# Order of SP's queue, ScalarE's copies and VectorE's low parts in the first tile of a fused attention and MLP kernel, and two sums of v moved to VectorE

## The chip, the cores and the metric

The kernel runs on one core of a Trainium2 chip. The metric is the device time of one execution in microseconds. Of three runs before the change the median is 788.79 us (787.68 to 790.22). A core has five engines with a queue each: TensorE (PE, matmuls and transposes), VectorE (DVE), ScalarE (ACT), GpSimd (POOL) and SyncE (SP), which here only issues DMAs. Each engine runs its queue in order; between engines there are only semaphores.

## The reference, cut to what matters

```python
q, k, v: (4, 8, 576, 64)                     # float32
q_d, k_d, v_d = means of 4 neighbouring rows # 144 pooled rows
out_d    = softmax(scale * q_d @ k_d.T) @ v_d
out_up   = repeat(out_d, 4, axis=2)
mask     = |i - j| < 4
out_local = softmax(where(mask, scale * q @ k.T, -1e9)) @ v
x = (out_up + out_local) as (2304 tokens, 512)
x = (x @ w_a) * (x @ w_b) @ w_out            # 512 -> 1536 -> 512
h = x @ w_in                                 # 512 -> 1024
solu = h * softmax(h)
y = layernorm(solu) * g_ln @ w_out2          # 1024 -> 512, the output
```

All is float32. Each product of the two MLPs is done as three matmuls on split operands: a high part (the value rounded by a copy to the type fp32r) and a low part (the value minus the high part): high x high, low x high, high x low.

## The kernel before, in words

The 2304 tokens are six tiles of 384. Tile m's block j (12 blocks of 128 of the 1536 middle columns) is: two up-products (kinds WA and WB, `up_product`, 12 matmuls each) of block j+1, and one down-product of block j (`down_product`, 12 matmuls into four PSUM banks that stay open through the tile). g = 12m + j counts blocks through all tiles. Between the products lie 36 gaps a tile, n = 3j, 3j+1, 3j+2 (`between(m, n)` exists on TensorE, ScalarE and VectorE): attention for tile m+1 is done in them piece by piece. `jobs_at` places the pooled attention: job i has scores at its first gap (`pooled_scores`), maximum on VectorE a gap later, exponentials on ScalarE two gaps later, a transposition three later (`turn_pooled`, copied by ScalarE's `pT_copy`), values four later (`pooled_values`, copied and stored by `out_d_copy`). In tile 0 job 0 starts at gap 0, job 1 at gap 5, so its values are due at gap 9. `local_at` places the local attention on VectorE: 17 steps a unit (7 products and reductions of q and k, the softmax, then products with v and sums; ScalarE does four of the v-parts, `unit_values`) and an END step, which writes `accT`; two units a tile, (1,0) and (1,1) in tile 0. `turns_at` places the four transpositions of the finished x (`turn_x`), in tile 0 at gaps 29, 30, 32 and 33. `QK_AT` places the pooling of raw q (gap 15) and raw k (gap 17) of the next batch, 48 small matmuls each.

What a block passes through: TensorE up(g,A) -> ScalarE `a_copy(g)` -> VectorE `gate(g)` once up(g,B) is done -> ScalarE `ab_high(g)` -> VectorE `ab_low(g)` (GpSimd in tiles 4 and 5) -> TensorE down(g). up(g,B) also needs gate(g-1), as they share a PSUM bank. W_out's block needs, in tile 0 and up to block 6 of tile 1, a DMA into one of three slots (`load_wo(g)`, free once down(g-3) is done), ScalarE's `wo_high(g)` and `wo_low(g)` (VectorE for blocks 0 and 1, GpSimd after). The weights W_a and W_b come in pairs of blocks (`load_weights(i)`, blocks 2i and 2i+1) and need ScalarE's `weight_high(j)` and `weight_low(j)` (VectorE for blocks 0 and 1, GpSimd after) in tile 0.

Ahead of tile 0 is the head: attention for tile 0 with nothing to hide it, for four pairs c of heads, on all engines: `head_local(c)` copies the local part to `x_raw`, `head_turn_pooled(c)` and `head_up(c)` do the pooled part, `head_x(c)` adds them, `x_high`, `x_low` split them. v_d, the pooled v of batch 0, comes from `raw_v` by `pool_v` on GpSimd, two additions of halves each, for the pairs in the order 1, 2, 3, 0. Then VectorE does the low parts of the first two blocks and the first two local steps, and `gate(0)`.

What sets the order around the change: every engine's queue is written out by hand, so an instruction that waits holds up all behind it. SP's queue (from `load_q_head` to `tile(m)`) issues nearly all DMAs; `tile(m)` puts loads at blocks j or gaps n, and many wait for semaphores first. `load_unit_v(1, 0)` overwrites `raw_v`, so it waits for all sums of v.

## Time and profile before

| | |
|---|---|
| median of 3 runs | 788.79 us (787.68 to 790.22) |
| the profiled execution | 785.7 us |
| its span, first to last instruction | 783.9 us |
| mean granted TensorE clock | 0.991 of full speed |
| TensorE busy | 762.2 us, 97% of the span |
| VectorE busy | 549.0 us, 70% |
| ScalarE busy | 299.0 us, 38% |
| GpSimd busy | 193.3 us, 25% |

Busy time is that of instructions on the engine; idle time of an engine matters only where another waits for it. The waits of an engine are listed with the instruction that released it; a wait for several semaphores goes to the one that came last, and "issue" is a wait of which the profile shows no releaser. Times are counted from the span's start. Matmuls overlap, so each shows about 0.33 us while they start 0.17 apart.

### The profile page before, as it was taken

How to read it: one execution, taken by the hardware profiler on the slowest of the kernel's cores; microseconds unless marked ns; L12 is line 12 of the kernel's file. 1: busy time of each engine (PE TensorE's matmuls, PEld its weight loads, DVE VectorE, ACT ScalarE, POOL GpSimd, SP SyncE). 2: the span in 40 equal slices, each digit the busy share in tenths (PEclk: the TensorE clock that was granted, in tenths of full speed). 3: DMA queues.
4: the chain of work that ended last, by engine and by line, in shares of the span. 5: the costliest groups of instructions: out<-in, count | busy, mean ns of one | idle time of the engine just before them, and what ended most of it. 6: DMA issues, size and time to landing. Idle time of an engine off the chain costs nothing.

```text
span 783.9 us, 12654 instructions
## 1 busy us (share of the span) xinstructions
PE 762.2 (97%) x4626; PEld 706.4 (90%) x4626; DVE 549.0 (70%) x978; ACT 299.0 (38%) x819; POOL 193.3 (25%) x244
## 2 busy tenths in 40 slices
PE   8997899898999999999999999999999999999998
PEld 7886899898999999999999999999988888888886
DVE  6796777979869887778777776122467766666663
ACT  4644537363353534344524424234322222222222
POOL 3656655355414330050001111122100000000000
PEclk9998999999999999999999999999999999999999
DMA  9999946586788575572746433636121011011011
GB/s 183 219 208 203 215 136 184 154 260 181 227 208 231 143 212 172 161 216 80 218 140 177 139 94 111 206 104 216 53 68 54 27 54 54 28 54 54 29 41 40
DMA packets 94650, 108.84 MB, mean 139 GB/s; under 512 B 29309, under 2 KB 62589, under 8 KB 94589
## 3 DMA queue, kind: packets, MB, share of 16 engines
q1 hardware_dynamic: 83293, 99.38, 48.3%
q10 hardware_dynamic: 11296, 8.65, 3.5%
q8 instruction: 37, 0.61, 0.3%
q14 instruction: 24, 0.20, 0.1%
HBM read 87.46 MB, written 20.55 MB: 138 GB/s over the span
## 4 chain that ended last, share of the span: by engine, by line
PE 91%; SPq 5%; DMA 1%; issue 1%; DVE 1%; ACT 0%; DVEq 0%; ACTq 0%
PE psum L931 28%; PE psum L933 27%; PE psum L932 27%; PE psum L1058 2%; SPq L503 2%; PE psum L888 2%; PE psum L841 1%; PE psum L865 1%; PE psum L899 1%; SPq L532 1%; DMA wo_raw<-in_moe_w_out 1%; PE psum L875 1%; SPq L557 1%; DMA v_h<-in_v 1%; SPq L469 1%
## 5 line engine op out<-in xcount | busy, mean ns | idle before, releaser
L931 PE MATMUL psum<-x_hi,w_hi 128*128 128x384 f32 x576 | 198.8, 345 | 0.6 <-DVE x_lo L1467 0.4
L933 PE MATMUL psum<-x_hi,w_lo 128*128 128x384 f32 x576 | 193.7, 336 | 0.0
L932 PE MATMUL psum<-x_lo,w_hi 128*128 128x384 f32 x576 | 193.5, 336 | 0.0
L1477 DVE TENSOR_TENSOR ab_f<-psum,a_sb 128x384 f32<-128x384 f32 x72 | 39.9, 554 | 104.4 <-PE psum L933 62.6
L931 PEld LDWEIGHTS psum<-x_hi,w_hi 128*128 128x128 f32 x576 | 109.0, 189 | 3.7 <-issue 3.3
L932 PEld LDWEIGHTS psum<-x_lo,w_hi 128*128 128x128 f32 x576 | 108.9, 189 | 0.0
L933 PEld LDWEIGHTS psum<-x_hi,w_lo 128*128 128x128 f32 x576 | 108.7, 189 | 0.0
L931 PE MATMUL psum<-ab_hi,wo_hi 128*128 128x384 f32 x288 | 100.9, 350 | 4.5 <-issue 4.5
L933 PE MATMUL psum<-ab_hi,wo_lo 128*128 128x384 f32 x288 | 97.7, 339 | 0.0
L932 PE MATMUL psum<-ab_lo,wo_hi 128*128 128x384 f32 x288 | 97.5, 339 | 0.0
L1817 POOL TENSOR_TENSOR ab_lo<-ab_f,ab_hi 128x384 fp32r<-128x384 f32 x24 | 29.5, 1229 | 182.6 <-ACT ab_hi L1229 182.6
L1510 DVE TENSOR_TENSOR tmp<-q_u,k_u 128x768 f32<-128x768 f32 x70 | 69.4, 994 | 3.7 <-DMA k_u<-in_k 3.6
L1224 ACT ACTIVATE a_sb<-psum 128x384 f32<-128x384 f32 x72 | 35.1, 487 | 85.4 <-PE psum L933 81.7
L1791 POOL TENSOR_TENSOR raw<-raw 96x256 f32<-96x256 f32 x42 | 40.4, 989 | 105.7 <-DMA raw<-in_q 49.9
L1519 DVE TENSOR_REDUCE p_u<-tmp 128x12 f32<-128x768 f32 x70 | 66.0, 942 | 0.1
L1229 ACT ACTIVATE ab_hi<-ab_f 128x384 fp32r<-128x384 f32 x72 | 37.5, 521 | 65.5 <-DVE ab_f L1477 59.5
L931 PEld LDWEIGHTS psum<-ab_hi,wo_hi 128*128 128x128 f32 x288 | 54.9, 190 | 6.9 <-issue 6.7
L1259 ACT ACTIVATE e_sb<-psum,neg_max 128x1024 f32<-128x1024 f32 x18 | 20.1, 1118 | 106.3 <-DVE neg_max L1681 106.3
L1869 POOL TENSOR_TENSOR rstd<-var_eps,exponent 128x1 f32<-128x1 f32 x18 | 9.9, 550 | 194.4 <-DVE var_eps L1703 194.4
L931 PE MATMUL psum<-w_hi,lnT_hi 128*128 128x512 f32 x144 | 57.6, 400 | 0.0
L933 PE MATMUL psum<-w_hi,lnT_lo 128*128 128x512 f32 x144 | 56.3, 391 | 0.0
L931 PE MATMUL psum<-win_hi,y_hi 128*128 128x512 f32 x144 | 56.1, 390 | 0.0
(157 smaller groups left out, 1427.6 us busy)
## 6 DMA issues: line engine op xcount, KB each, us to landing
wo_hi<-wo_hi_scratch SPq DMA_DIRECT2D x53, 256.0 KB, 2.7
wo_lo<-wo_lo_scratch SPq DMA_DIRECT2D x53, 256.0 KB, 3.1
wo_raw<-in_moe_w_out SPq DMA_DIRECT2D x19, 256.0 KB, 4.7
yT_scratch<-y_sb ACTq DMA_DIRECT2D x6, 768.0 KB, 5.9
y_raw<-yT_scratch SPq DMA_DIRECT2D x18, 256.0 KB, 2.9
out<-out_sb SPq DMA_DIRECT2D x18, 256.0 KB, 2.1
k_u<-in_k SPq DMA_DIRECT2D x11, 384.0 KB
v_u<-in_v SPq DMA_DIRECT2D x11, 384.0 KB
```

Source lines behind the costliest of these rows:

```text
L503: sp.dma_start(paired_rows(t)[:, :, x, :], bass.AP(src.tensor, b * H * S * D + half * 3 * R4 * D + x * PPB * S * D, [[6 * R4 * D, PPB * BL ...
L931: mm(dst, wh, xh, start=first, stop=False, skip_group_check=not check)
L932: mm(dst, wh, xl, start=False, stop=False, skip_group_check=not check)
L933: last = mm(dst, wl, xh, start=False, stop=end, skip_group_check=not check)
L1224: A(a_sb[:, g % 2, :], bank(GA, NT), ACT.Copy).then_inc(s.a_copied, 1)
L1229: A(ab_hi[:, g % 2, :], ab_f[:, g % 2, :], ACT.Copy).then_inc(s.ab_hi_ready, 1)
L1259: A(e_sb[:, par, :], psum[:, HB[par][0] * BANK:HB[par][0] * BANK + F2], ACT.Exp, bias=neg_max[:, par:par + 1], accum_out=e_sum[:, par:par ...
L1477: V.tensor_tensor(ab_f[:, g % 2, :], bank(GB, NT), a_sb[:, g % 2, :], ALU.mult).then_inc(s.ab_ready, 1)
L1510: last = V.tensor_tensor(tmp[:, step % 3], q_u[:, :, :], k_u[:, :, step * D:step * D + TPP * D], ALU.mult)
L1519: last = V.tensor_reduce(p_u[:, step - 1, :], tmp[:, (step - 1) % 3] .rearrange("p h (t d) -> p (h t) d", d=D), AX.X, ALU.add)
L1791: last = G.tensor_tensor(t[:, :, i, 0:128], t[:, :, i, 0:128], t[:, :, i, 128:256], ALU.add)
L1817: G.tensor_tensor(ab_lo[:, g % 2, :], ab_f[:, g % 2, :], ab_hi[:, g % 2, :], ALU.subtract).then_inc(s.ab_lo_by_pool, 1)
```

## The change

In words, by engine:

- SP: after `load_unit_v(1, 0)`, which now waits for two sums of GpSimd and two of VectorE, `load_weights(3)` and `load_wo(3)` are issued ahead of raw q (they were in tile 0's block 1). `load_weights(4)` and `(5)` go to blocks 2 and 4, behind `load_wo` of the block; unit (1,1)'s q and k go from gap 11 to 9, its v from gap 19 to 16; the store of pooled v and the load of raw k go from block 3 to gap 10; `load_vd(1)` from gap 10 to 13.
- VectorE: `sum_v(1)` and `sum_v(0)`, two reductions each, in the head; the head's last steps interleaved in another order; in all tiles `ab_low(g)` ahead of the gap 3j; in tile 0 the local steps of gaps 16 on run faster and end at gap 27 rather than 29.
- ScalarE: `weight_high(0)` ahead of `head_pooled_pT(2)`; in all tiles `a_copy(g+1)` ahead of gap 3j+1, and `wo_high(g+1)` behind gap 3j+2; in tile 0 `weight_high` by the table `SPLIT_AT`, blocks 8 and 9 in j = 6, 10 and 11 in j = 7.
- GpSimd: `pool_v` for pairs 2 and 3 only; `weight_low` by the same table.
- TensorE: `head_turn_pooled(3)` ahead of `head_up(1)`; waits on sums of v split by who makes them.

```diff
--- before.py
+++ after.py
@@ -97,8 +97,8 @@
         if m == 0:
-            todo = 2 * STEPS - FIRST
-            first, end = FIRST + n * todo // 30, FIRST + (n + 1) * todo // 30
+            first, end = (FIRST + i * 16 // 15 if i < 16 else 19 + (i - 16) * 4 // 3 for i in (n, n + 1))
         else:
@@ -108,6 +108,9 @@
+SPLIT_AT = {0: (2,), 2: (4,), 3: (5,), 4: (6,), 5: (7,), 6: (8, 9), 7: (10, 11)}
...
@@ -596,8 +599,11 @@
-            sp.wait_ge(s.v_summed, PPB)
+            sp.wait_ge(s.v_summed, 2)
+            sp.wait_ge(s.v_by_vector, 2)
             load_unit_v(1, 0)
+            load_weights(3)
+            load_wo(3)
             load_raw(1, 0, 0)
@@ -606,24 +612,19 @@
                         store_wo(g)
-                    if m == 0 and j in (1, 3, 5):
-                        load_weights((j + 5) // 2)
-                    if m == 0 and j == 3:
-                        store_vd(1, 0)
-                        store_vd(1, 1)
-                        load_raw(1, 1, 0)
-                        load_raw(1, 1, 1)
-                    if g + SLOTS - 1 < FC * TILES and (m > 0 or j > 0):
+                    if g + SLOTS - 1 < FC * TILES and (m > 0 or j > 1):
                         load_wo(g + SLOTS - 1)
+                    if m == 0 and j in (2, 4):
+                        load_weights(j // 2 + 3)
                     for n in range(3 * j, 3 * j + 3):
...
                             rest = m in (0, 3)
-                            if n == (11 if m == 0 else 4):
+                            if n == (9 if m == 0 else 4):
                                 load_unit_q(m + 1, 1)
...
                                 load_xup(m + 1, 0)
-                            if n == (19, 14, 14, 20, 14)[m]:
+                            if n == (16, 14, 14, 20, 14)[m]:
                                 load_unit_v(m + 1, 1)
@@ -650,7 +651,12 @@
             def pooling(m, n):
-                if (m, n) in ((0, 10), (3, 10)):
+                if m == 0 and n == 10:
+                    store_vd(1, 0)
+                    store_vd(1, 1)
+                    load_raw(1, 1, 0)
+                    load_raw(1, 1, 1)
+                if (m, n) in ((0, 13), (3, 10)):
                     load_vd(1 if m == 0 else 3)
@@ -807,8 +813,10 @@
                     pe.wait_ge(s.raw_v_loaded, 32)
+                elif c == 1:
+                    pe.wait_ge(s.v_by_vector, 1)
                 else:
-                    pe.wait_ge(s.v_summed, c)
+                    pe.wait_ge(s.v_summed, c - 1)
                 if c == 0:
@@ -879,7 +887,8 @@
                 if JOBS[i][3] == 0:
-                    pe.wait_ge(s.v_summed, PPB)
+                    pe.wait_ge(s.v_summed, 2)
+                    pe.wait_ge(s.v_by_vector, 2)
                 else:
@@ -1029,8 +1038,8 @@
             head_turn_pooled(2)
+            head_turn_pooled(3)
             head_up(1)
-            head_turn_pooled(3)
             head_up(2)
@@ -1292,8 +1301,8 @@
             head_pooled_exp(3)
+            weight_high(0)
             head_pooled_pT(2)
-            weight_high(0)
             head_pooled_pT(3)
@@ -1308,14 +1317,15 @@
                     between(m, 3 * j)
-                    if m == 0 and j != 1 and j + HEAD_BLOCKS < FC:
-                        weight_high(j + HEAD_BLOCKS)
-                    between(m, 3 * j + 1)
+                    if m == 0:
+                        for i in SPLIT_AT.get(j, ()):
+                            weight_high(i)
                     if g + 1 < FC * TILES:
                         a_copy(g + 1)
+                    between(m, 3 * j + 1)
+                    between(m, 3 * j + 2)
                     if g > 0 and g + 1 < FC * TILES and wo_fresh(g + 1):
                         wo_high(g + 1)
-                    between(m, 3 * j + 2)
                     if g == 0:
@@ -1439,6 +1449,15 @@
+            def sum_v(c):
+                dve.wait_ge(s.raw_v_loaded, 32)
+                for x in range(2):
+                    last = V.tensor_reduce(v_d[:, c, x, :].rearrange("p (y d) -> p y d", y=2),
+                                           raw_v[:, x, :, c, :].rearrange("p y (r d) -> p y d r", r=R4),
+                                           AX.X, ALU.add)
+                last.then_inc(s.v_by_vector, 1)
             def head_local(c):
@@ -1502,7 +1521,8 @@
-                        dve.wait_ge(s.v_summed, PPB)
+                        dve.wait_ge(s.v_summed, 2)
+                        dve.wait_ge(s.v_by_vector, 2)
                         dve.wait_ge(s.q_loaded, 16 * loads_to(u, 0, TPP))
@@ -1632,22 +1652,24 @@
             head_pooled_max(3)
-            head_local(3)
+            sum_v(1)
             head_pooled_norm(2)
             head_pooled_norm(3)
+            head_local(3)
             head_x(0)
+            weight_low(0, WA)
             head_x(1)
-            weight_low(0, WA)
             x_low(0, 0)
             head_x(2)
+            x_low(0, 1)
             head_x(3)
-            x_low(0, 1)
-            weight_low(0, WB)
             x_low(0, 2)
             x_low(0, 3)
+            weight_low(0, WB)
             wo_low(0)
...
                 weight_low(1, kind)
+            sum_v(0)
             wo_low(1)
@@ -1656,9 +1678,9 @@
                     g = FC * m + j
-                    between(m, 3 * j)
                     if m < LOW_BY_POOL:
                         ab_low(g)
+                    between(m, 3 * j)
                     between(m, 3 * j + 1)
@@ -1834,7 +1856,7 @@
                 normalise(c)
-            for i, c in enumerate((1, 2, 3, 0)):
+            for i, c in enumerate((2, 3)):
                 pool_v(i, c)
@@ -1843,8 +1865,9 @@
                         ab_low(g)
-                    if m == 0 and 2 <= j < FC - HEAD_BLOCKS:
-                        weight_low(j + HEAD_BLOCKS)
+                    if m == 0 and j > 1:
+                        for i in SPLIT_AT.get(j, ()):
+                            weight_low(i)
                     if g > 0 and g + 1 < FC * TILES and wo_fresh(g + 1):
```

## Rows read from the trace of the kernel before

**Rows 1.** The page, busy us of each engine, its share and instructions.

```profile
PE 762.2 (97%) x4626; PEld 706.4 (90%) x4626; DVE 549.0 (70%) x978; ACT 299.0 (38%) x819; POOL 193.3 (25%) x244
```

**Rows 2.** TensorE's waits, 0 to 180: total us, times, longest us.

```profile
PE psum L888 <- ACT pT_pool L1155: 5.4, 1, 5.4
PE psum L899 <- DVE accT L1574: 2.6, 1, 2.6
PE psum L931 <- issue: 2.4, 1, 2.4
...
PE psum L825 <- ACT pT_head L1138: 1.0, 1, 1.0
```

**Rows 3.** Windows: length, busy of each engine (instructions), clock, DMA share, GB/s.

```profile
37.70:49.20 11.50, 11.12 (x72) 10.36 (x71) 11.50 (x18) 5.60 (x12) 3.47 (x5) 1.00 1.09 199
...
66.70:89.80 23.10, 15.28 (x89) 14.88 (x90) 15.69 (x13) 12.11 (x36) 16.20 (x19) 0.85 0.96 193
89.80:141.40 51.60, 51.60 (x363) 49.30 (x361) 38.39 (x53) 26.74 (x68) 29.70 (x33) 1.00 0.60 161
```

**Rows 4.** TensorE's timeline: start, us, line, tiles; in brackets idle before it.

```profile
47.10 0.33 PE L931 MATMUL psum<-x_hi,w_hi 128*128 128x384 f32 x1
...
49.18 0.33 PE L931 MATMUL psum<-ab_hi,wo_hi 128*128 128x384 f32 x1
...
184.41 0.41 PE L931 MATMUL psum<-ab_hi,wo_hi 128*128 128x384 f32 x1 [2.13 <-issue]
...
185.36 0.52 PE L933 MATMUL psum<-ab_hi,wo_lo 128*128 128x384 f32 x1
```

**Rows 5.** Chain of waits, pieces in order: start us, us, what.

```profile
73.86 0.32 PE psum L932
...
76.10 0.23 PE psum L933
...
144.53 0.32 PE psum L931
...
147.74 0.26 PE psum L932
```

**Rows 6.** ScalarE's timeline.

```profile
34.28 1.04 ACT L1203 ACTIVATE w_hi<-w_raw 128x1024 fp32r<-128x1024 f32 x1
...
70.95 0.63 ACT L1208 ACTIVATE wo_hi<-wo_raw 128x512 fp32r<-128x512 f32 x1 [8.36 <-DMA wo_raw<-in_moe_w_out]
```

**Rows 7.** SP's timeline of DMA issues; last, raw q from issue to landing.

```profile
47.43 13.07 SPq L503 DMA_DIRECT2D raw<-in_q  x4
...
64.20 1.08 SPq L541 DMA_DIRECT2D wo_raw<-in_moe_w_out  x2
...
84.73 1.72 SPq L557 DMA_DIRECT2D q_u<-in_q  x4
...
DMA to landing us min/median/max: 6.2/10.6/14.3
```

**Rows 8.** VectorE's groups, 66 to 142: busy us, mean ns, idle before.

```profile
L1550 DVE TENSOR_TENSOR tmp<-v_u,p_u 128x768 f32<-128x768 f32 x6 | 8.7, 1464 | 0.0
...
L1519 DVE TENSOR_REDUCE p_u<-tmp 128x12 f32<-128x768 f32 x7 | 6.6, 944 | 0.1
```

**Rows 9.** VectorE's timeline.

```profile
44.71 0.94 DVE L1519 TENSOR_REDUCE p_u<-tmp 128x12 f32<-128x768 f32 x1
45.57 0.54 DVE L1477 TENSOR_TENSOR ab_f<-psum,a_sb 128x384 f32<-128x384 f32 x1
...
61.98 3.01 DVE L1535 TENSOR_SCALAR u_den<-u_sum 128x12 f32<-128x12 f32 x1
...
86.43 1.07 DVE L1481 TENSOR_TENSOR ab_lo<-ab_f,ab_hi 128x384 fp32r<-128x384 f32 x1
...
182.00 2.31 DVE L1481 TENSOR_TENSOR ab_lo<-ab_f,ab_hi 128x384 fp32r<-128x384 f32 x1
```

**Rows 10.** GpSimd's timeline.

```profile
73.03 3.85 POOL L1791 TENSOR_TENSOR raw<-raw 96x256 f32<-96x256 f32 x3
```

More of the change, by code:

```diff
@@ L385, in build_program @@
         names = w_names + wo_names + wos_names + raw_names + qh_names + kh_names + """v_h_loaded q_loaded k_loaded v_loaded
-        xup_loaded xup_stored0 xup_stored1 raw_v_loaded v_step v_summed vd_stored0 vd_stored1 vd_loaded y_stored win_loaded w2_loaded g_loaded y_loaded0
+        xup_loaded xup_stored0 xup_stored1 raw_v_loaded v_step v_summed v_by_vector vd_stored0 vd_stored1 vd_loaded y_stored win_loaded w2_loaded g_loaded y_loaded0
         y_loaded1 out_stored0 out_stored1
```

## The prediction, made before the changed kernel ran

> **What bounds the kernel now.** The page first: TensorE is busy 762.2 of 783.9 us [rows 1], so whatever is not on its path is free, and only about 22 us of the span, plus slow-clock time, can be won at all. So the second view is the table of what TensorE waited for, up to 180 us. It has four entries that matter [rows 2]: 5.4 us for `pT_pool`, a copy by ScalarE; 2.4 us put down to "issue"; 2.6 us for `accT`, an addition by VectorE; 1.0 us for `pT_head`. The timeline adds a fifth of 2.13 us in tile 1, at 184.41 [rows 4]. All five lie in stretches whose order the change rewrites. Below, tile 0's block j is up-products for block j+1 (kinds A and B), then down-product j; n = 3j, 3j+1, 3j+2 are the gaps.
>
> The third view is the windows. From 66.70 to 89.80 TensorE is busy 15.28 of 23.10 us at a mean granted clock of 0.85, and at 1.00 from 89.80 to 141.40, where it never stops [rows 3]. At full speed (2.4 GHz) the twelve matmuls of up(1,B), 47.10 to 49.18, take 2.08 us, 0.173 each [rows 4]. The first window holds up(4), down(3), up(5), down(4): 24+12+24+12 = 72 matmuls, 12.5 us, and the sixteen small ones of pooled_values (0.65 at full speed, as at 53.89). So 23.10 - 13.15 = 9.95 us are lost there: 5.43 and 2.40 in waits, 2.1 in matmuls at the 1.2 GHz level after the long wait (0.32 apart until 76.10 [rows 5]).
>
> The fourth view names the cause. ScalarE sits 8.36 us before `wo_hi` at 70.95, released by the DMA of `wo_raw`; `pT_pool` comes right behind it at 71.49 [rows 2, 6]. That DMA is W_out of block 3, issued only at 64.20, because SP spent 47.43 to 60.50 issuing raw q and then the weights [rows 7]. So TensorE waits for a copy that needs nothing from W_out, and only stands behind it in ScalarE's order.
>
> **The change part by part** (minus is faster).
>
> 1. Head. weight_high(0), 1.04 us at 34.28 [rows 6], stands before the copy `pT_head` that TensorE waits 1.0 for [rows 2]; now it runs in ScalarE's idle time of 2.17 us ahead of 33.9. Then, in VectorE's new order with its own durations (1.1 for a norm, 0.5 for local, head_x and x_low, 0.6 for a w_lo or wo_lo, start to start): norm(3) done at 33.4, local(3) 33.9, head_x(0) 34.4, w_lo(0,WA) 35.1, and by turns head_x and x_low until the last x_low at 38.7. TensorE, with turn(3) ahead of up(1), is through the head's ups at 36, so up(0,A) ends near 39.3 where it ended at 41.9. But the next gate belongs to VectorE, which is busy without a break there, and two sum_v are added. Price of sum_v: not in this trace. Bounds: two reductions of 512 input elements; the nearest row is 944 ns for 768 [rows 8], so 0.63 each; from below 1.15 a pair, since the next instruction starts 0.86 after such a reduction (44.71 to 45.57 [rows 9]); from above 2.0, if they are slowed as products beside GpSimd are (1464 against 944 [rows 8]). I take 1.25, by the reductions' own row. sum_v(1) fills a 1.2 us hole; sum_v(0) is on the path. From 38.7 VectorE has w_lo(0,WB), wo_low(0) and two w_lo of block 1, to 41.1; sum_v(0), 42.3; wo_low(1), 42.9; two products and a reduction, 2.7, so gate(0) stays at 45.6 to 46.05 [rows 9]: what it saved in the head, it adds. up(1,B) needs that gate: it starts at 46.1 instead of 47.10. Gain 1.0 of the 2.6; the rest becomes a wait of 1.8 us there, the size after which the clock sometimes fell for some ten matmuls (2.13 at 184.41 did it, 2.4 at 85 did not); half of 1.5: +0.8. Bounds of the head: -2.5 to +1.5.
> The Trainium skill (SBUF — State Buffer, section "Who interferes with whom") says that a VectorE instruction with two SBUF inputs contends with a GpSimd instruction that reads SBUF, and a tensor_reduce never does. By that rule sum_v keeps the lower price beside GpSimd's own sums, and the sum stands; without it 0.75 is added for sum_v(0). The 944 against 1464 agrees.
>
> 2. The wait of 5.43. pT_copy(1) goes ahead of wo_high(3); weights 3 and W_out 3 go ahead of raw q in SP's queue. Weights 3 issue from 47.4, W_out 3 waits for down(0), now at 50.2, and lands near 62.5 rather than 70.95. pT_copy(1) then needs only the turn at 63. The wait goes, and with it the slow clock.
>
> 3. The wait of 2.40 at 87.60. VectorE's ab_lo of block 4 runs at 86.43 for 1.07 [rows 9], behind a local step, and down(4) starts as it ends. Now ab_low(g) precedes the steps. The wait goes. So 2 and 3 give 9.95.
>
> What is late next: VectorE worked 15.69 us in that window [rows 3], and TensorE now wants to be through in 13.15. So up to 2.5 us of new waits, and nothing if the steps slip into the 10.7 us of TensorE's turns of raw at n = 15 and 17, for which VectorE has no due work. The other candidate is GpSimd: its sums of raw v, 3.85+1.3 us [rows 10], stand before weight_low(5), whose ScalarE copy is now due near 70; W_lo(5,A) is there at 71.7 to 73.5, TensorE wants it at 72. These overlap. +1.3 (0 to 2.5).
>
> 4. Raw q starts 5 us later and has landed near 71 (before: 59.4+6.2 = 65.6 [rows 7]); TensorE turns it at 79.5, before 89.8. Raw k goes after store_vd, about 78, lands by 86, wanted near 89. Slack 3 us: cost nothing; if the store of half 1 waits for GpSimd's sums to 75, still 0 to 1. Weights 4 and 5 move up; splitting blocks 8 to 11 in pairs at j = 6, 7 puts 5.8 us in front of GpSimd's wo_low, which is due a whole block (6 to 7 us) later: 0 to 1, taken 0.
>
> 5. The wait of 2.6 for `accT` at 141. From 89.8 to 141.4 VectorE works 38.39 of 51.60 us [rows 3], so it is not short of time, only its last steps (n = 28, 29) stand too late. They now end at n = 27, and v is loaded three gaps earlier. -2.6, and -1.6 for eleven matmuls at half rate (0.32 apart from 144.53 to 147.74 [rows 5]; 11 x 0.146). Needs unit (1,1) to start on time: q and k of it are issued at 69 to 73 instead of from 84.73 [rows 7].
>
> 6. Tile 1, 184.41. ab_lo runs at 182.00 for 2.31 us [rows 9] behind two steps; ahead of them it could begin at 179.3. -2.13 and -1.5 for the ten slow matmuls from 185.36 to 188.56 [rows 4]; but the steps then stand before gate at 186.5, due at 186.2: +0.8. In tiles 2 and 3 the same reorder meets no wait above 0.6: nothing.
>
> Sum: -1.0 + 0.8 - 9.95 + 1.3 - 2.6 - 1.6 - 2.1 - 1.5 + 0.8 = -15.9. The profiled execution took 785.7 us (span 783.9 and 1.8 around it), so 769.8 on its own footing; the median of the runs is 788.79, 3.1 above it. On that footing 772.9, so 773.
>
> **Rivals.**
> - A, the waits come back smaller (20 in 100). VectorE and GpSimd slow each other, so the new waits reach their bound in 3 (2.5) and also 4 (1), and 5 and 6 give nothing, since accT and ab_lo are still behind. -1.0+0.8-9.95+3.5 = -6.65: 782.1. For: 15.69 against 13.15; products at 1464 ns. For, too: a TENSOR_SCALAR of 12 numbers took 3.01 us at 61.98, GpSimd being busy [rows 9]. Against: 13 us of idle time of VectorE in the window after.
> By the Trainium skill (SBUF — State Buffer, same section) the loser of that port is blocked for the whole instruction, so each added overlap would cost up to a whole operation of GpSimd; that is this rival's mechanism, and 1464 against 944 agrees that the products are slowed.
> - B, the wait only moves (7 in 100). Had W_out 3 still not landed by down(3), at 69.75, because DMA serves the same bytes ahead of it, ScalarE's block stands one step later, and TensorE waits 5.4 there with 2.1 of slow clock again, and raw k, behind it, costs what 5 and 6 bring: -1.0+0.8-9.95+7.5+1.3 = -1.35, 787.4, no change. Against: 1.1 MB of 256-byte pieces now lie behind it, not ahead.
> - C, slower (8 in 100). VectorE becomes TensorE's pace in tile 0: ab_low(g) now stands in front of its steps and waits for ScalarE's ab_hi uncovered, so every gate is late. Price a block: 2.1 of wait and 1.5 of half-rate matmuls, as at 184.41. It turns the sign from 15.9/3.6 = 4.4 blocks; at six (blocks 2 to 7) +21.6: 794.5. For: VectorE has no idle time at all from 37.70 to 49.20 [rows 3]. Against: by step 5's window blocks 6 to 11 have slack, and six late gates would have to come from there too.
>
> **Numbers.** My forecast holds 65 in 100, its own range 768 to 778 (head -2.5 to +1.5, new waits 0 to 2.5, tile 1 to -3.6). With A most of the way the range is 767 to 783. A difference under 0.3% (2.4 us) can't be told from none. Faster 0.84, within 0.07, slower 0.09.
>
> **What would show it.** Right: no wait of TensorE above 2 us before 130; `wo_hi` of block 3 near 64 without DMA idle; gate(0) still near 46 with TensorE idle about 1.8 us before up(1,B); turns of raw at 79 to 80 rather than 89.8; no `accT` wait at the change of tile; granted clock near 1.0 in every window to 180. Wrong: idle time before up(·,B) in several blocks of tile 0 (C), `wo_raw` releasing ScalarE late (B), TensorE waiting for raw k at n = 17, sum_v above 2 us.

## The result and the profile after

The changed kernel takes 781.79 us (median of 8 runs, 778.01 to 783.32) against 788.0 (8 runs, 785.75 to 791.68). The ratio is 0.9909, 95% interval 0.9882 to 0.9936: 5 to 9 us faster, where 16 were forecast. In the two profiled executions 785.7 became 780.66, the span 783.9 became 778.9. Both traces cover the same 4626 matmuls.

The page of the changed kernel, in the columns of [rows 1]:

```profile
PE 760.4 (98%) x4626; PEld 703.4 (90%) x4626; DVE 554.3 (71%) x982; ACT 299.0 (38%) x819; POOL 193.6 (25%) x236
```

TensorE's waits up to 180 us made 11.4 us in four rows [rows 2] and one in the timeline [rows 4]. This is the same view of the changed kernel (to 200 us; total us, times, longest us). Its L940 to L942 are L931 to L933 of before, L873 is the scores of a pooled job, L908 `turn_x`:

```profile
PE psum L940 <- DVE x_lo L1489: 1.8, 1, 1.8
PE psum L940 <- DVE ab_f L1496: 1.7, 1, 1.7
PE psum L940 <- POOL w_lo L1825: 1.5, 1, 1.5
PE psum L908 <- DVE accT L1594: 1.4, 2, 0.8
PE psum L873 <- ACT out_d L1173: 1.4, 1, 1.4
...
PE psum L940 <- DVE ab_lo L1500: 0.9, 1, 0.9
PE psum L940 <- POOL wo_lo L1833: 0.9, 1, 0.9
```

The 5.4, the 2.4 and the 2.13 are gone. `accT` fell from 2.6 in one place to 1.4 in two, 0.8 at the change of tile and 0.7 in tile 1. In their stead stand five waits that were not there, of 0.9 to 1.7 each, and x_lo, 0.2 before, is 1.8. The windows, cut where TensorE begins the same work as in [rows 3] (up to down(0); pooled_values(1) to the turns of raw q; to down(9); to the end of down(15)):

```profile
37.70:50.03 12.33, 10.66 (x68) 9.78 (x67) 11.62 (x18) 5.37 (x9) 0.71 (x1) 1.00 1.09 199
67.27:83.50 16.23, 13.78 (x89) 12.84 (x88) 16.16 (x15) 11.13 (x35) 16.05 (x18) 1.00 1.05 239
83.50:134.80 51.30, 47.88 (x338) 45.08 (x338) 42.73 (x56) 24.99 (x65) 34.82 (x34) 1.00 0.68 168
134.80:181.08 46.28, 44.43 (x262) 42.66 (x261) 36.09 (x53) 20.88 (x63) 19.94 (x21) 0.96 0.70 206
```

The second row is the core of it. The work that took 23.10 us takes 16.23, at full clock. But VectorE is busy 16.16 of these and GpSimd 16.05: there is almost no idle time left on either. The third row begins with the turns of raw q, at 83.50, where the prediction had 79.5.

The start of each down-product, read from TensorE's timelines, says where the lead was won and lost (not rows of a view; us, minus is ahead of before):

```
down(g)   g=0    2    3     4     5     7     9    10    11    15    16    18
before  49.18 64.34 78.80 87.60 104.61 120.46 134.58 144.28 152.98 184.41 193.29 207.07
changed +0.85 +0.85 -6.44 -6.08 -6.11 -4.62 -1.99 -4.75 -3.11 -5.41 -7.03 -5.98
```

| stretch | step of the prediction | forecast | measured |
|---|---|---|---|
| head, to down(0) | 1 | -0.2 | +0.85 |
| to down(4) | 2 and 3, with the new waits | -8.65 | -6.93 |
| down(4) to down(9) | 4 | 0 | +4.1 |
| down(9) to down(11) | 5 | -4.2 | -1.1 |
| down(11) to down(18) | 6 | -2.8 | -2.9 |
| from there to the end | none | 0 | +1.0 |
| sum | | -15.9 | -5.0 |

### The profile page after: what moved, and what is told of

Its sections match the earlier page's. It is cut to its first block, busy times and chain, and to the rows that moved or that the text cites. A ratio compares the mean times of both kernels' runs of the same rounds, so it can differ in the third digit from the quotient of the medians.

```text
span 778.9 us, 12652 instructions
## 1 busy us (share of the span) xinstructions
PE 760.4 (98%) x4626; PEld 703.4 (90%) x4626; DVE 554.3 (71%) x982; ACT 299.0 (38%) x819; POOL 193.6 (25%) x236
## 3 DMA queue, kind: packets, MB, share of 16 engines
q10 hardware_dynamic: 11296, 8.65, 3.6%
## 4 chain that ended last, share of the span: by engine, by line
PE 78%; POOL 2%; DMA 1%; ACT 0%; issue 0%; SPq 0%; DVE 0%; DVEq 0%
PE psum L940 24%; PE psum L942 24%; PE psum L941 24%; PE psum L1067 2%; PE psum L897 1%; PE psum L873 1%; DMA raw<-in_q 1%; POOL raw L1813 1%; PE psum L908 1%; POOL raw L1817 1%; PE psum L883 1%; PE psum L855 0%; ACT out_sb L1359 0%; ACT out_d L1173 0%; SPq L547 0%
## 5 line engine op out<-in xcount | busy, mean ns | idle before, releaser
L940 PE MATMUL psum<-x_hi,w_hi 128*128 128x384 f32 x576 | 198.8, 345 | 5.0 <-DVE x_lo L1489 1.8
L942 PE MATMUL psum<-x_hi,w_lo 128*128 128x384 f32 x576 | 193.6, 336 | 0.0
L940 PEld LDWEIGHTS psum<-x_hi,w_hi 128*128 128x128 f32 x576 | 108.7, 189 | 8.9 <-issue 6.4
L942 PEld LDWEIGHTS psum<-x_hi,w_lo 128*128 128x128 f32 x576 | 108.7, 189 | 0.0
L940 PE MATMUL psum<-ab_hi,wo_hi 128*128 128x384 f32 x288 | 99.6, 346 | 1.8 <-DVE ab_lo L1500 0.9
L942 PE MATMUL psum<-ab_hi,wo_lo 128*128 128x384 f32 x288 | 96.6, 335 | 0.0
L1813 POOL TENSOR_TENSOR raw<-raw 96x256 f32<-96x256 f32 x42 | 42.5, 1036 | 104.3 <-DMA raw<-in_q 51.2
L940 PEld LDWEIGHTS psum<-ab_hi,wo_hi 128*128 128x128 f32 x288 | 54.1, 188 | 4.1 <-issue 4.0
L940 PE MATMUL psum<-w_hi,lnT_hi 128*128 128x512 f32 x144 | 57.6, 400 | 0.0
L942 PE MATMUL psum<-w_hi,lnT_lo 128*128 128x512 f32 x144 | 56.3, 391 | 0.0
L940 PE MATMUL psum<-win_hi,y_hi 128*128 128x512 f32 x144 | 56.1, 390 | 0.0
```

What stands on the lines that cost most here:

```text
L940: mm(dst, wh, xh, start=first, stop=False, skip_group_check=not check)
L942: last = mm(dst, wl, xh, start=False, stop=end, skip_group_check=not check)
L1813: last = G.tensor_tensor(t[:, :, i, 0:128], t[:, :, i, 0:128], t[:, :, i, 128:256], ALU.add)
```

## The experiments

All ratios are to the kernel before, with 95% intervals; the changed kernel's is 0.9909 [0.9882, 0.9936]. "Lead" is the start of a down-product against the kernel before, in the profiled execution. The head by itself ends up to 3 us earlier or later from one execution to another: with the changed kernel's head down(0) lies at -0.15 to +3.09 in six traces, with the head of before at -0.39 to +2.73 in six. So leads are read as differences between two down-products of one trace, and "loses 3.0" means that the later one is 3.0 less ahead.

**One part undone at a time**

Local steps of tile 0 as before:

```diff
-            first, end = (FIRST + i * 16 // 15 if i < 16 else 19 + (i - 16) * 4 // 3 for i in (n, n + 1))
+            todo = 2 * STEPS - FIRST
+            first, end = FIRST + n * todo // 30, FIRST + (n + 1) * todo // 30
```

> The changed kernel with one part undone: the local steps of tile 0 are placed as before (the last at gap 29, not 27). Theory S (the denser steps of gaps 16 to 27 make VectorE late, and ScalarE's exponential, due at gap 21 rather than 23, blocks out_d): the waits for out_d (1.4) and GpSimd's wo_lo (0.9) at 113 to 124 go, but the accT wait at gap 32 comes back to some 2.6; together 1 us faster to 1 us slower than the changed kernel, so 778 to 783. Rival O (the steps are no burden, VectorE is late because it waits uncovered for ab_hi): the waits at 113 to 124 stay, accT comes back, 2 to 4 us slower, 784 to 786.

Measured: 779.09 us, 0.9909 [0.9877, 0.9942]. From down(5) to down(11) it gains 0.7, where the changed kernel loses 3.0; the waits for out_d and wo_lo are gone and accT's is 2.0. So theory S holds for the mechanism. VectorE still waits as long for ab_hi as in the changed kernel (4.00 there):

```profile
102.54 0.79 DVE L1501 TENSOR_TENSOR ab_lo<-ab_f,ab_hi 128x384 fp32r<-128x384 f32 x1 [4.02 <-ACT ab_hi L1239]
```

Yet down(4) to down(9) loses 0.4 instead of 4.1. The other traces agree: with the denser steps it loses 4.1 in the changed kernel and in four variants of it (all sums of v on GpSimd, the neighbours' sum, the sums of raw v earlier, x_low first), 3.5 and 2.0 in the two others; with the old steps it loses 0.3 to 0.4 in all four traces that have them. In the time it is not shown: the ratios are the same, and the medians differ by 2.7, with a head 2.2 us later in this trace.

ab_low behind the gap again:

```diff
-                    if m < LOW_BY_POOL:
-                        ab_low(g)
                     between(m, 3 * j)
+                    if m < LOW_BY_POOL:
+                        ab_low(g)
```

> The changed kernel with one part undone: ab_low(g) stands behind gap 3j again, in all tiles. Theory O (ab_low ahead makes VectorE idle, 4.0 us at 96 and 2.6 at 116, and these are the waits of gaps 22 to 31): the four waits between 110 and 135, 4.1 us, become under 1.5, but the wait before down(4) (2.4 before the change, 0.9 in the changed kernel) and the one of 2.1 with its slow clock in tile 1 return: 0 to 3 slower in sum, 782 to 785. Rival S: the waits between 110 and 135 stay as they are, and the sum is 4 to 6 slower, 786 to 788.

Measured: 781.68, 0.9930 [0.9896, 0.9964]. From down(5) to down(11) it gains 1.1, where the changed kernel loses 3.0, but not in every part of it: down(7) to down(9) still loses 2.0, for a wait of 1.6 for wo_lo. And TensorE comes to this stretch 3.4 us later against the kernel before than in the changed kernel, as it waited 4.0 for w_lo(5), so VectorE had more time. Theory O is half borne out and not shown apart from that. The wait of 4.0 need not be the price of this edit either, as the next run has it without the edit. No difference in the sum.

Weight blocks 8 to 11 one at a time:

```diff
-SPLIT_AT = {..., 6: (8, 9), 7: (10, 11)}
+SPLIT_AT = {..., 6: (8,), 7: (9,), 8: (10,), 9: (11,)}
```

> The changed kernel with one part undone: weight blocks 8 to 11 are split one each in j = 6 to 9 (as the kernel before did), not in pairs at j = 6 and 7. Theory W (two weight_high in a row hold up out_d at 114.3 by 1 us, eight subtractions of GpSimd hold up wo_lo until 124): the waits for out_d and wo_lo, 2.3 us, fall under 0.8; 1.5 to 2.5 faster than the changed kernel, 779 to 780. Rival (ScalarE waits 2.6 us for VectorE there anyway): under 0.5 of difference.

Measured: 780.18, 0.9914 [0.9883, 0.9945]; the waits for out_d and wo_lo went, but accT's grew to 3.4, and down(5) to down(9) still lost 3.5 (changed kernel: 4.1). Theory W fell as to the gain. This trace differs from the changed kernel's before block 6, where both have the same program: down(3) to down(4) loses 4.2 instead of 0.4, for a wait of 4.0 on w_lo(5). What VectorE and GpSimd (below it) do there:

```profile
75.16 8.23 DVE L1578 TENSOR_TENSOR tmp<-tmp,part 128x768 f32<-128x768 f32 x1
```

```profile
76.33 2.79 POOL L1825 TENSOR_TENSOR w_lo<-w_raw,w_hi 128x256 fp32r<-128x256 f32 x4
79.09 1.41 POOL L1833 TENSOR_TENSOR wo_lo<-wo_raw,wo_hi 128x256 fp32r<-128x256 f32 x2
80.47 3.52 POOL L1825 TENSOR_TENSOR w_lo<-w_raw,w_hi 128x256 fp32r<-128x256 f32 x4
```

An addition that takes 0.94 while GpSimd is idle stays 8.23 us on VectorE, to 83.39, while GpSimd ends a sum and runs ten subtractions without a gap. So the size of the wait for w_lo(5) varies between executions of one order: 1.5 to 1.6 in the changed kernel, with the old steps and with x_low first, 4.0 here.

All sums of v on GpSimd (the counts that others wait for go with it, not shown here or below):

```diff
-            sum_v(1)
-            sum_v(0)
-            for i, c in enumerate((2, 3)):
+            for i, c in enumerate((1, 2, 3, 0)):
```

> The changed kernel with one part undone: all four sums of v on GpSimd again, in the order 1, 2, 3, 0. Theory V (the two sums on VectorE cost 2.0 us each in its queue, twice the term I used, and the second delays gate(0) by 2.0): gate(0) starts near 45.3 rather than 47.2, TensorE waits under 0.3 before up(1,B), 1.5 to 2 us faster at down(0); in the end, as later waits take part of it, 0.5 to 2 faster, 780 to 781. Rival (GpSimd's sums slow VectorE's head by as much): gate(0) above 46.5, no difference.

Measured: 780.39, 0.9921 [0.9893, 0.9948]. The wait of 1.7 before up(1,B) is gone, and down(0) is 2.5 us ahead of the changed kernel's, more than the wait and within what the head varies by itself. By down(4) it is 0.9 behind, with 3.6 of wait for w_lo(5). Theory V holds for the place; in the time nothing shows.

**The price of a sum**

```diff
-  raw_v[:, x, :, c, :].rearrange("p y (r d) -> p y d r", r=R4)
+  raw_v[:, x, :, c, :].rearrange("p y (d r) -> p y d r", r=R4)
```

> The changed kernel, its two sums of v reading four neighbouring values of a row instead of four values 64 apart (so pooled v of two pairs is another sum; the count of elements and everything else is the same). Theory R (the reduction's price is set by the distance of its inner elements, 256 bytes): 0.6 to 0.65 us a reduction instead of 1.0, and gate(0) 0.8 us earlier. Rival (72 partitions and 512 elements cost 1.0 in any order; or GpSimd slows it): 1.0 us again.

Measured (VectorE's timeline, two reductions):

```profile
41.42 1.27 DVE L1456 TENSOR_REDUCE v_d<-raw_v 72x128 f32<-72x512 f32 x2
```

0.63 us each against 1.01, and the wait before up(1,B) falls from 1.7 to 0.9. It has one run, 779.43, and its pooled v is another sum, so only the durations are used. Theory R holds: 512 elements cost what the row of 768 says only if the four that are summed lie side by side; 256 bytes apart they cost 1.6 times that.

**Easing what is late**

GpSimd's sums of raw v one place earlier:

```diff
             weight_low(3)
+            pool_rows(1, 2, 0)
...
-                    if m == 0 and j in (1, 2):
-                        pool_rows(1, 2, j - 1)
+                    if m == 0 and j == 1:
+                        pool_rows(1, 2, 1)
```

> The changed kernel with one thing moved: GpSimd's sums of raw v of batch 1 come one place earlier (half 0 before block 0's loop, half 1 at block 1), into its idle time, so that none stands before weight_low(5). Theory G (the sum of half 1 holds up w_lo(5), for which TensorE waits 1.5 in the changed kernel's profile and 3.6 to 4.0 in three of the variants'): that wait falls under 0.5 and down(4) starts 8 to 10 us before where it did before the change, against 6.1; half of it reaches the end, 1 to 3 us faster than the changed kernel, 779 to 781. Rival P (VectorE and GpSimd block each other there whatever GpSimd does, so w_lo(5) is late as before): no difference.

Measured: 782.29, 0.9923 [0.9903, 0.9944]. TensorE still waits for w_lo, 2.6 us in three places, the longest 1.7. Theory G fell: no difference.

The same, pair 0's sum on GpSimd, local steps as before:

```diff
+            pool_rows(1, 2, 0)      # as above
-            sum_v(0)
-            for i, c in enumerate((2, 3)):
+            for i, c in enumerate((2, 3, 0)):
+            first, end = ...        # the local steps as before
```

> The changed kernel with three edits: sums of raw v earlier as in the other run, the sum of v's pair 0 by GpSimd in its idle time (VectorE keeps pair 1), the local steps of tile 0 placed as before the change. Theory D (each of VectorE's and GpSimd's late due times in tile 0 costs what it shows, and they add up when all are eased): before up(1,B) no wait (1.7 in the changed kernel), before up(5,A) under 0.5 (1.5), gaps 22 to 31 under 1 (4.1 us lost): 4 to 6 us faster than the changed kernel, 776 to 778. Rival (the next wait is always right behind, as unit (1,1)'s steps or the stores of pooled output bound the tile's end): 779 to 781.

Measured: 779.14, 0.9895 [0.9856, 0.9933]. No wait before up(1,B), none in gaps 22 to 26; but w_lo costs 2.1, accT 2.0, x_lo 2.1. The rival described it: the next wait is right behind.

And x_low ahead of the local steps:

```diff
             def between(m, n):          # VectorE
...
-                local_steps(m, n)
                 if n in turns_at(m):
                     x_low(m + 1, turns_at(m)[n])
+                local_steps(m, n)
```

> As the run with three edits, and at the turns of x VectorE does x_low ahead of the local steps of the same gap, in all tiles. Theory D: x_lo of the last pair is what up(12,A) waits 1.8 for, with 1.4 of slow clock behind it; both go, 2 to 3.5 us faster than the run with three edits, 773 to 776. Rival: the wait is ScalarE's x_high or the transposition's accT, not the order on VectorE; no difference.

Measured: 773.46 us (773.24 to 775.34), 0.9818 [0.9795, 0.9842]: the best of all. Its interval and that of the next run are the only ones that lie clear of the changed kernel's. Its waits from 38 to 400 us, and below them VectorE's and ScalarE's timeline around the one for w_lo(5):

```profile
PE psum L941 <- POOL w_lo L1825: 2.5, 3, 1.7
...
PE psum L941 <- DVE x_lo L1490: 0.8, 1, 0.8
```

```profile
68.19 3.29 DVE L1431 TENSOR_SCALAR pool_den<-pool_sum 128x2 f32<-128x2 f32 x1
```

```profile
71.77 0.52 ACT L1174 ACTIVATE out_d<-psum,pool_inv 128x64 f32<-128x64 f32 x2 [2.94 <-DVE pool_inv L1434]
...
75.09 1.05 ACT L1213 ACTIVATE w_hi<-w_raw 128x1024 fp32r<-128x1024 f32 x1
```

x_lo fell from 2.1 to 0.8. The wait for w_lo(5) has a chain that a table of waits does not show: `pool_den`, two numbers a partition, is 3.29 us on VectorE while GpSimd splits block 4; ScalarE waits 2.94 of them for its result before out_d; behind out_d, its stores and a unit of values stands weight_high(5), at 75.09.

weight_high ahead of the gap, on top of it:

```diff
                     ab_high(g)
+                    if m == 0:
+                        for i in SPLIT_AT.get(j, ()):
+                            weight_high(i)
                     between(m, 3 * j)
```

> As the run with x_low ahead of the local steps, and in tile 0 ScalarE does weight_high ahead of gap 3j, so that block 5's no longer stands behind out_d, its two stores and a unit of values. Theory D (w_lo(5) is late because weight_high(5) is, at 75.1, while it could be done at 70; TensorE waits 1.7 us for it there): that wait goes, 1 to 2.5 us faster, 771 to 773. Rival (VectorE and GpSimd block each other, w_lo(5) is only pushed into another wait): the same 773 to 774.

Measured: 774.35, 0.9852 [0.9825, 0.9878]. weight_high(5) runs at 66.84 and the waits for w_lo(5) go; of the 2.5 for w_lo 0.4 is left, ahead of them. But another of 2.4 stands at down(3), as the same two numbers a partition now take 6.08 us on VectorE, from 65.25, and stand before ab_lo(3). The rival was right: the wait moved, and the time did not fall.

The same edit of x_low (the diff two above), by itself on the kernel before:

> The kernel before, with one edit: at the turns of x VectorE does x_low ahead of the local steps of the same gap, in all tiles. In its own profile the wait for x_lo at the change of tile is 0.2 us. Theory N (that wait is the next behind those that the change took away, and had no price before it): within 1.5 us of the kernel before, 786.5 to 788.5. Rival (the order costs 3 us in every tile whatever stands before it): 3 to 6 faster, 782 to 785.

Measured: 787.9, 1.0013 [0.9996, 1.0030]. By itself on the changed kernel:

> The changed kernel, with one edit: at the turns of x VectorE does x_low ahead of the local steps of the same gap, in all tiles. The same edit gave nothing on the kernel before (ratio 1.0013). Theory N (with the waits ahead of it gone, x_lo at the change of tile holds TensorE for 1.8 us and the clock falls behind it): 2.5 to 4 faster than the changed kernel, 777 to 779. Rival (it needs the old placing of the local steps too): under 1 of difference.

Measured: 778.65, 0.9891 [0.9857, 0.9926]; down(9) to down(11) gains 3.7 instead of 1.1, the wait for x_lo falls from 1.8 to 0.8, the clock stays at 1.0. Worth nothing on the kernel before and 2.6 us in the trace of this one: theory N holds for the traces. But only 1.0 of the 2.6 is the wait. The rest is the clock, and behind an x_lo wait of 1.8 to 2.1 it fell in four traces (changed kernel, all sums of v on GpSimd, the neighbours' sum, the run with three edits) and stayed in three (old steps, one block each, sums of raw v earlier). The medians differ by 3.1, their intervals overlap.

**Parts of the change alone, on the kernel before**

ScalarE's order:

```diff
-                    between(m, 3 * j + 1)
                     if g + 1 < FC * TILES:
                         a_copy(g + 1)
+                    between(m, 3 * j + 1)
+                    between(m, 3 * j + 2)
                     if g > 0 and g + 1 < FC * TILES and wo_fresh(g + 1):
                         wo_high(g + 1)
-                    between(m, 3 * j + 2)
```

> The kernel before, with ScalarE's order of the change alone (a_copy ahead of gap 3j+1, wo_high behind gap 3j+2, in all tiles). Theory Q (pT_copy behind wo_high is the whole of the 5.4 us wait; the late DMA of W_out of block 3 then holds only down(3)): that DMA still lands near 70.9, and down(3), wanted at 71.2, starts near 73: 4 to 6 us ahead of the kernel before at down(3), 3 to 5 us at the end, 783 to 785. Rival (the queue of SP is the cause, ScalarE's order does nothing without it): TensorE waits 3 us or more at down(3) and at down(4), the end 0 to 2 faster, 786 to 788.

Measured: 784.97, 0.9974 [0.9956, 0.9992]. Its pT_copy runs at 67.41, ahead of wo_high(3) at 71.63, which waits for its DMA as before. SP's order (the whole of its queue in the change's diff, of which this is the core):

```diff
             load_unit_v(1, 0)
+            load_weights(3)
+            load_wo(3)
...
-                    if m == 0 and j in (1, 3, 5):
-                        load_weights((j + 5) // 2)
```

> The kernel before, with SP's order of the change alone (weights 3 and W_out of block 3 ahead of raw q, and the later loads as in the change). Theory Q (W_out of block 3 lands at 66.5 as in the changed kernel, so the copy behind it comes 4 us earlier, but still behind it): the wait at pooled_values becomes 1 to 2 us, down(3) 5 us ahead of the kernel before, 3 to 5 at the end, 783 to 785, about what ScalarE's order alone gives, and the two together are worth hardly more than one. Rival: the new order delays the loads of raw k and of unit (1,1) so that it gives nothing, 787 to 789.

Measured: 786.57, 0.9981 [0.9954, 1.0008]. Waits of TensorE, 38 to 400 us, of ScalarE's order alone and of SP's alone:

```profile
PE psum L931 <- POOL w_lo L1803: 5.4, 3, 4.5
...
PE psum L931 <- DVE x_lo L1470: 1.6, 1, 1.6
```

```profile
PE psum L933 <- issue: 8.5, 2, 6.4
```

Either takes the wait of 5.4: down(3) moves ahead by 7.3 and 7.0 against down(0). And either loses it on the next two down-products, 5.1 to w_lo(5), or 8.6 to waits of 6.4 and 2.1 that the profile puts down to no releaser. VectorE's rows name the 6.4, at down(4), 86.98:

```profile
74.70 4.33 DVE L1552 TENSOR_TENSOR tmp<-v_u,p_u 128x768 f32<-128x768 f32 x1
78.96 5.59 DVE L1560 TENSOR_TENSOR tmp<-tmp,part 128x768 f32<-128x768 f32 x1
...
86.33 0.55 DVE L1483 TENSOR_TENSOR ab_lo<-ab_f,ab_hi 128x384 fp32r<-128x384 f32 x1
```

Two steps that take 0.95 each from 84.58 on stay 9.9 us together, while GpSimd splits weights without a gap from 74.73 to 83.73, and ab_lo(4) stands behind them. Theory Q was right on the place and wrong on the end. Both together:

> The kernel before, with ScalarE's and SP's order of the change together, and nothing else of it. Each alone moved down(3) 7 us ahead and had given 5 to 7 of it back at down(4) or down(5). Theory H (what takes it back is VectorE's and GpSimd's order, which neither touches: ab_lo(4) behind the local steps, w_lo(5) behind the sums of raw v): down(3) 7 ahead again, by down(5) under 2.5 of it left, 1 to 3.5 us faster than the kernel before, 784 to 787. Rival J (the two only work together, and are the whole change: 6 to 7 us at down(5)): 780 to 782.

Measured: 783.13, 0.9930 [0.9903, 0.9956]. 7.3 ahead at down(3) against down(0), 3.8 left at down(5). More is kept than by either, which neither theory priced; H is the nearer. VectorE's order alone:

```diff
-                    between(m, 3 * j)
                     if m < LOW_BY_POOL:
                         ab_low(g)
+                    between(m, 3 * j)
```

> The kernel before, with ab_low(g) ahead of gap 3j alone, in all tiles. Theory H: the wait of 2.4 at down(4) and that of 2.1 in tile 1 with its slow clock go, the 5.4 stays; as VectorE had 4.2 us of idle time just before, nothing takes the gain back: 3.5 to 6 faster, 782 to 784. Rival (ab_low ahead leaves VectorE idle, its steps late, and accT's wait of 2.6 grows as much): 0 to 2 faster.

Measured: 786.69, 0.9977 [0.9961, 0.9994]. down(3) to down(4) gains 1.6; in tile 1, down(14) to down(15) gains 2.3, and 1.9 is gone by down(16) for a wait of 2.0 on p_pool. The rival's size, by another wait than it named.

Read across the traces, the gain of step 6 has another cause than the prediction gave it. From down(14) to down(16) the changed kernel gains 3.94; with ab_low back behind the gap it gains 3.95, with ScalarE's order alone on the kernel before 3.95, with ab_low ahead alone 0.43. VectorE with ScalarE's order alone, to be held against 182.00 in [rows 9]:

```profile
174.42 0.37 DVE L1420 TENSOR_SCALAR pool_den<-pool_sum 96x2 f32<-96x2 f32 x1
...
179.04 1.07 DVE L1481 TENSOR_TENSOR ab_lo<-ab_f,ab_hi 128x384 fp32r<-128x384 f32 x1
```

ab_lo(15) still stands behind the two steps, but comes 3.0 earlier; `pool_den` took 1.48 in the kernel before, at 174.88, and GpSimd is idle here for the 2.00 us up to 176.77, where it worked without a break before. Why the order of ScalarE's copies leaves it idle there was not isolated.

## Why the prediction was wrong

What bounds the kernel: right. The waits named were the ones that went, and that pT_copy only stood behind wo_high(3) is shown by ScalarE's order alone. W_out of block 3 let its copy begin at 66.77 rather than near 64, which cost TensorE nothing. The wrong part is what comes next. The step that failed is step 4, which put the stretch from down(4) to down(9) at nothing: it lost 4.1, and 3.7 of that goes with the local steps' new places, which step 5 credited and nothing priced. Step 5 failed with it, and the head and "what is late next" were mis-sized.

Step 1, the head, -0.2 forecast, +0.85 measured, less apart than the head varies by itself. Its order gave 1.05 us at the end of up(0,A) of the 2.6 forecast. Two things were mis-sized. The sums (VectorE's timeline of the changed kernel; then TensorE's at up(1,B)):

```profile
42.06 2.00 DVE L1456 TENSOR_REDUCE v_d<-raw_v 72x128 f32<-72x512 f32 x2
...
47.19 0.54 DVE L1496 TENSOR_TENSOR ab_f<-psum,a_sb 128x384 f32<-128x384 f32 x1
...
73.49 4.10 DVE L1578 TENSOR_TENSOR tmp<-tmp 128x768 f32<-128x768 f32 x1
...
100.35 0.80 DVE L1500 TENSOR_TENSOR ab_lo<-ab_f,ab_hi 128x384 fp32r<-128x384 f32 x1 [4.00 <-ACT ab_hi L1238]
```

```profile
47.88 0.41 PE L940 MATMUL psum<-x_hi,w_hi 128*128 128x384 f32 x1 [1.67 <-DVE ab_f L1496]
```

2.00 us against my 1.25, from the row of a reduction whose elements are neighbours; 2.0 had been my upper bound, for another reason. gate(0) came at 47.19, not 45.6, and 1.67 of wait stood there: up(1,B) started at 47.88, not 46.1. The clock did not fall after it, so the 0.8 for that was not needed.

"What is late next", +1.3 (0 to 2.5): measured 1.5 + 0.9 in the changed kernel's waits, 4.0 for w_lo(5) alone in the variant that has its program up to block 6, and 3.6 and 4.0 in two that differ from it in the sums of v or in ab_low. So the 2.4 of the changed kernel, inside the range, is partly luck. The reason given was right and underpriced. GpSimd, in its timeline:

```profile
68.87 3.88 POOL L1813 TENSOR_TENSOR raw<-raw 96x256 f32<-96x256 f32 x3
72.83 1.89 POOL L1817 TENSOR_TENSOR raw<-raw 96x128 f32<-96x128 f32 x3
74.68 3.51 POOL L1825 TENSOR_TENSOR w_lo<-w_raw,w_hi 128x256 fp32r<-128x256 f32 x4
```

The sums of half 1 take 5.8 us to 74.68, not 5.1, and w_lo(5) starts 1.7 us after its copy ends at 72.96. Running the sums earlier did not help, so they are not the whole cause but one of several loads on a pair of engines that have next to no idle time, as the window shows. VectorE's row at 73.49 is the same: 4.10 us for an addition of 0.94. I had named this as rival A. Its 782.1 is the time that came, but by luck and not by its own sum: it had step 6 at nothing, which came in full, and step 4 at +1.

Step 4, 0 (at most 1): measured +4.1, the largest error. I priced data, and they were in time: raw q and k held up nothing. What had no price anywhere is the denser local steps, for which step 5 only took credit. With the old steps this stretch loses 0.3 to 0.4. The other thing not priced is that ab_low(g) ahead of the steps waits uncovered: VectorE's row at 100.35 has 4.00 us of idle time, for an ab_hi that ScalarE could not do as it stood behind the copies of raw k. Rival C had that mechanism and looked for it at the gates. By itself it costs next to nothing here: the old steps have the same wait, 4.02, and ab_low ahead alone on the kernel before loses nothing from down(4) to down(9). Whether the denser steps need it to do their harm is open, as with ab_low behind the gap 2.0 is still lost. The steps of gaps 16 on came on a VectorE that was late, and ScalarE's exponential, now at gap 21, waited for them (ScalarE's timeline):

```profile
66.77 0.63 ACT L1217 ACTIVATE wo_hi<-wo_raw 128x512 fp32r<-128x512 f32 x1 [0.64 <-DMA wo_raw<-in_moe_w_out]
...
71.91 1.05 ACT L1212 ACTIVATE w_hi<-w_raw 128x1024 fp32r<-128x1024 f32 x1
...
111.90 0.27 ACT L1193 ACTIVATE p_u<-p_u 128x84 f32<-128x84 f32 x1 [2.63 <-DVE p_u L1549]
...
114.34 0.51 ACT L1173 ACTIVATE out_d<-psum,pool_inv 128x64 f32<-128x64 f32 x2
```

2.63 us before `p_u` at 111.90, two weight copies behind it, and out_d at 114.34, 3.0 after TensorE had its values at 111.31: the wait of 1.4. The pairs of weight copies are not the cause by themselves, as one block each still lost 3.5.

Step 5, -4.2: measured -1.1. What the move of the local steps bought there is 0.9 to 1.6, read between pairs of traces that differ in it and in edits ahead of this stretch, and in which the clock did the same (0.9 with x_low first, 1.6 in two other pairs), against the 3.7 that it cost from down(4) to down(9). The `accT` wait shrank and its slow clock went, but the turn of the tile had a second queue position of the same kind. x_lo of the last pair stood behind a local step of the next unit, and cost 1.8 and then ten matmuls at the 1.2 GHz level, 146.13 to 149.33 in the chain of waits:

```profile
145.10 0.41 PE psum L940
...
146.13 0.32 PE psum L941
...
149.01 0.32 PE psum L941
149.33 0.18 PE psum L942
```

The step failed where it said that only the last local steps stood too late. The 0.2 that the kernel before waited for x_lo was this one, as I read it, hidden by the accT wait ahead of it. x_low ahead of the steps takes 1.0 of the 1.8, and with no slow matmuls behind it this stretch gains 3.7.

Step 6 was right in size, -2.9 for -2.8, and wrong in cause. It gave the gain to ab_low ahead of the steps, but ScalarE's order alone gives it, and ab_low back behind the gap keeps it. Its +0.8 came too, though not at the gate: down(16) to down(17) loses 0.84, for a wait of 0.65 for accT. Both are luck.

On the whole: the shares of busy time (15.69 of 23.10, 38.39 of 51.60) gave slack as a sum. Around the wait of 5.4 VectorE sat idle 4.2 us and GpSimd 6.0, in the kernel before:

```profile
72.51 0.97 DVE L1481 TENSOR_TENSOR ab_lo<-ab_f,ab_hi 128x384 fp32r<-128x384 f32 x1 [4.17 <-ACT ab_hi L1229]
```

```profile
71.66 1.41 POOL L1811 TENSOR_TENSOR wo_lo<-wo_raw,wo_hi 128x256 fp32r<-128x256 f32 x2 [6.01 <-ACT wo_hi L1208]
```

That this idle time was the slack is argued, not isolated; the three runs that took the wait away with nothing else for VectorE or GpSimd changed lost 5.1 of 7.3, 8.6 of 7.0 and 3.5 of 7.3 within two down-products. The best variant, 0.9818, shows that 14 of the 16 us were there to be had, with four orders more altered (two of them back to the kernel before). What it would take to free TensorE between down(2) and down(4) in that variant is not settled: with w_lo(5) out of the way another wait came, and which VectorE instruction is held up beside GpSimd, and how long, varies from execution to execution. The 1.0 lost behind down(18) was not looked into, but for a wait of 0.8 on GpSimd's sum of raw.

## What to carry to other kernels

Before crediting a removed wait, list for each other engine what it did in that wait: idle time there may be slack that the next stretch was living on, and it goes with the wait. Then go through the new order instruction by instruction, pricing each wait that nothing covers, and each instruction that stands behind a step of a later unit, since busy shares do not show either. A step moved earlier has a price as well as a gain. And when a term of the sum comes out right, undo its cause by itself before believing it. A reduction's price must be read from a row with the same distance between the elements that are summed.

## What the runs showed of the hardware

- A reduction of 512 elements a partition, on 72 partitions of float32, takes 0.63 us when the four summed are adjacent and 1.01 when they lie 256 bytes apart.
- When GpSimd runs subtractions back to back, a VectorE instruction is not only slowed from 0.94 to 1.48: one stayed 8.23 us, until GpSimd's tenth had nearly ended, and a TENSOR_SCALAR on two numbers a partition 3.29 and 6.08 (in the changed kernel, at 68.06, 0.17, though GpSimd works there too). The Trainium skill (SBUF — State Buffer, section "Who interferes with whom") says that of VectorE and GpSimd the loser of the shared port pair is blocked for the other's whole instruction. By that, with GpSimd's instructions of 0.7, one lost turn would have cost a tenth of the wait that was measured. The rows look as if it lost ten times in a row, and where they and the rule differ they decide.
- The reductions beside GpSimd's work kept their price (944 ns a mean in [rows 8]; 2.04 and 2.00 a pair of sums in the changed kernel, the first beside GpSimd's own, the second with GpSimd idle).
